# Turning the first expert stage's hidden rows in 32 by 32 blocks on VectorE, with weight sets released in two steps

## The reference, cut to what matters

```python
expert_idx = np.argmax(x @ w_gate, axis=1)      # 8 experts
for e in range(8):
    xe = x[expert_idx == e]
    h = np.maximum(xe @ w1[e], 0.0)             # 512 -> 1024
    out[mask] = gate_w[mask, None] * (h @ w2[e])  # 1024 -> 512
```

## Time and profile before

| | us |
|---|---|
| three runs | 1193.3, 1193.42, 1194.82 |
| median | 1193.42 |
| the profiled execution's own time | 1194.6 |
| its span | 1193.0 |
| PE busy | 1129.5 (95%) |
| DVE busy | 704.5 (59%) |
| ACT busy | 583.6 (49%) |
| POOL busy | 257.4 (22%) |

### The profile page before, as it was taken

The page is one execution under the profiler, slowest core; times in us unless marked ns, Lnnn a source line. Parts: engine busy times, 40 slices in busy tenths (PEclk is TensorE's granted clock), DMA queues, the critical chain, the costliest instruction groups (busy, mean ns, idle before and its releaser), DMA issues.

```text
span 1193.0 us, 19326 instructions
## 1 busy us (share of the span) xinstructions
PE 1129.5 (95%) x6205; PEld 930.1 (78%) x6206; DVE 704.5 (59%) x1373; ACT 583.6 (49%) x1041; POOL 257.4 (22%) x184
## 2 busy tenths in 40 slices
PE   5999899839999999999999999999999999999996
PEld 4777777738888888888887787888888888888885
DVE  5788788741111111111124997986986986986974
ACT  5767576512222222222234765665665665665662
POOL 1101111135255646637250000100100100100101
PEclk9999899969999999999999999999999999999999
DMA  9997851157377767858473001001001001000000
GB/s 184 304 223 180 213 139 57 43 196 248 116 255 229 246 221 248 262 179 284 157 274 126 1 1 37 36 1 36 35 0 36 35 0 36 35 0 1 36 1 35
DMA packets 138136, 141.44 MB, mean 119 GB/s; under 512 B 100448, under 2 KB 100448, under 8 KB 137056
## 3 DMA queue, kind: packets, MB, share of 16 engines
q0 software_dynamic: 27584, 92.48, 22.5%
q1 hardware_dynamic: 110496, 48.26, 16.2%
HBM read 117.65 MB, written 23.32 MB: 118 GB/s over the span
## 4 chain that ended last, share of the span: by engine, by line
PE 79%; DVE 12%; issue 3%; ACT 3%; DMA 2%; POOL 1%; SPq 0%; POOLq 0%; DVEq 0%; ACTq 0%
PE bank L955 21%; PE bank L957 21%; PE bank L956 21%; PE bank L806 3%; PE bank L843 3%; PE bank L819 2%; PE bank L986 2%; PE bank L787 2%; PE bank L859 2%; DVE poly L1499 1%; DVE gl L1521 1%; DVE poly L1497 1%; PE bank L950 1%; DVE prob L1166 1%; DVE quot_b L1491 1%
## 5 line engine op out<-in xcount | busy, mean ns | idle before, releaser
L441 POOL TENSOR_TENSOR w_lo<-stage,w_hi 128x2048 fp32r<-128x2048 f32 x32 | 147.3, 4603 | 55.5 <-DMA w_hi<-in_moe_w_dram 18.2
L955 PE MATMUL bank<-w_hi,gh 128*128 128x512 f32 x384 | 150.6, 392 | 2.4 <-DVE gl L1521 2.4
L955 PE MATMUL bank<-x2Th,w_hi 128*128 128x512 f32 x384 | 149.6, 390 | 1.9 <-ACT ybuf L666 1.4
L957 PE MATMUL bank<-w_hi,gl 128*128 128x512 f32 x384 | 149.5, 389 | 0.0
L956 PE MATMUL bank<-w_lo,gh 128*128 128x512 f32 x384 | 149.4, 389 | 0.0
L957 PE MATMUL bank<-x2Th,w_lo 128*128 128x512 f32 x384 | 149.4, 389 | 0.0
L956 PE MATMUL bank<-x2Tl,w_hi 128*128 128x512 f32 x384 | 149.4, 389 | 0.0
L558 POOL DMA_INDIRECT out_dram<-stage,ids x24 | 28.5, 1187 | 521.8 <-ACT stage L746 504.9
L1414 DVE TENSOR_TENSOR hTl<-bank,hTh 128x512 fp32r<-128x512 f32 x62 | 39.9, 685 | 151.8 <-ACT hTh L671 151.8
L1408 DVE TENSOR_TENSOR xTl<-bank,xTh 128x512 fp32r<-128x512 f32 x31 | 21.4, 691 | 159.3 <-ACT xTh L659 159.3
L955 PE MATMUL bank<-w_hi,xTh 128*128 x248 | 100.2, 404 | 2.3 <-DVE xTl L1408 1.6
(11 more groups left out here) (204 smaller groups left out, 2325.6 us busy)
## 6 DMA issues: line engine op xcount, KB each, us to landing
w_hi<-in_moe_w_dram POOLq DMA_DIRECT2D x32, 1024.0 KB, 5.9
stage<-in_moe_w_dram POOLq DMA_DIRECT2D x32, 1024.0 KB, 8.2
xg<-routed_x SPq DMA_DIRECT2D x31, 256.0 KB, 2.7
routed_y<-ybuf SPq DMA_DIRECT2D x31, 256.0 KB, 5.4
x<-routed_y SPq DMA_DIRECT2D x6, 1056.0 KB, 5.1
kraw<-in_k_dram SPq DMA_DIRECT2D x24, 256.0 KB, 4.3
qraw<-in_q_dram SPq DMA_DIRECT2D x24, 256.0 KB, 5.1
vraw<-in_v_dram SPq DMA_DIRECT2D x24, 256.0 KB, 5.6
```

What stands on the lines that cost most here:

```text
L441: pool.tensor_tensor(w_lo[:, at:at + CH], stage[:, c % 2, :], w_hi[:, at:at + CH].bitcast(F32), ALU.subtract).then_inc(chunk_ready, 1)
L955: pe.matmul(dst, lhs_hi, rhs_hi, start=first, stop=False)
L957: return pe.matmul(dst, lhs_lo, rhs_hi, start=False, stop=last)
```

## The change

It takes the eight transposes of `hbuf` away from PE for tiles 0 to 29. DVE turns `hbuf` instead, in blocks of 32 by 32, into a tile `hT` in SBUF (it lies where `poly` of the dense layer lies). One instruction reads 32 partitions and 8 blocks of 32 columns and writes 32 partitions, and 16 of them turn a tile, eight (`turn_h(t, 0)`) for rows 0 to 63 and eight for rows 64 to 127. DVE's x step of the next tile stands between the two groups. `hTh` and `hTl` are formed from `hT` in two halves by rows instead of from the PSUM banks in two halves by columns. The last tile is turned on PE as before. PE's up has two new waits: before it writes a bank of `H_ps`, the Relu of the tile before has read it. ACT's Relu has one: `hbuf` has been turned.

POOL's wait before a set is cut in two. `up_free` waits on `h_ps` for the up product of the last tile of the old expert, `down_free`, behind the first split, on `tile_done` for the down product.

```diff
-            def half_free(e):
-                n = pool.value_load(end_i[0:1, ds(e, 1)], min_val=1, max_val=MT + 1)
+            def up_free(e):
+                n = pool.value_load(end_i[0:1, 1, ds(e, 1)], min_val=2, max_val=2 * MT)
+                pool.wait_ge(h_ps, n)
+                settle(pool)
+            def down_free(e):
+                n = pool.value_load(end_i[0:1, 0, ds(e, 1)], min_val=2, max_val=MT + 1)
                 pool.wait_ge(tile_done, n)
                 settle(pool)

+                if old is not None:
+                    up_free(old)
                 cast_in(0, par, srcs, kinds)
                 cast_in(1, par, srcs, kinds)
                 for c in range(4):
                     split(s, c, par)
+                    if c == 0 and old is not None:
+                        down_free(old)
                     if c < 2:
                         cast_in(c + 2, par, srcs, kinds)

             def moe_ht(t):                                   # ACT
-                for n in range(2):
-                    act.wait_ge(ht_ps, 2 * t + n + 1)
-                    act.activation(hTh[:, 4 * n:4 * n + 4, :], HT_ps[n][:, :].rearrange("p (j n) -> p j n", j=4),
-                                   ACT.Copy).then_inc(ht_hi, 1)
+                for k in range(2):
+                    cols = slice(64 * k, 64 * k + 64)
+                    act.wait_ge(h_turned, 2 * t + k + 1)
+                    act.activation(hTh[:, :, cols], hT[:, :, cols], ACT.Copy).then_inc(ht_hi, 1)

                 for n in range(2):                           # PE, moe_up
+                    if not isinstance(t, int) or t > 0:
+                        pe.wait_ge(h_sb, 2 * t + n - 1)

                 moe_down(t - 1, off_down, e_down)            # PE, pe_tile
-                moe_turn_h(t)
                 moe_up(t + 1, off_up, e)

+            def turn_h(t, k):                                # DVE
+                if not isinstance(t, int) and k == 0:
+                    dve.wait_ge(ht_lo, 2 * t)
+                dve.wait_ge(h_sb, 2 * t + 2)
+                for q in (2 * k, 2 * k + 1):
+                    for r in range(4):
+                        rows = hbuf[q * QD:(q + 1) * QD, :].rearrange("p (j r i) -> p j r i", r=4, i=QD)[:, :, r, :]
+                        ins = dve.transpose(hT[r * QD:(r + 1) * QD, :, q * QD:(q + 1) * QD], rows)
+                ins.then_inc(h_turned, 1)

             def moe_ht(t):                                   # DVE
-                    dve.tensor_tensor(hTl[:, 4 * n:4 * n + 4, :], HT_ps[n][:, :].rearrange("p (j n) -> p j n", j=4),
-                                      hTh[:, 4 * n:4 * n + 4, :].bitcast(F32), ALU.subtract).then_inc(ht_lo, 1)
+                    dve.tensor_tensor(hTl[:, :, cols], hT[:, :, cols], hTh[:, :, cols].bitcast(F32),
+                                      ALU.subtract).then_inc(ht_lo, 1)

-            with dve.Fori(0, MT - 1) as t:
-                moe_x(t + 1); moe_ht(t)
+            turn_h(0, 0); moe_x(1); turn_h(0, 1); moe_ht(0)
+            with dve.Fori(1, MT - 1) as t:
+                turn_h(t, 0); moe_x(t + 1); turn_h(t, 1); moe_ht(t)
```

More of the change, by code:

```diff
@@ L18 @@
 E, F = 8, 1024
+QD = 32
 F2 = 2048
@@ L96, in build_program @@
         dest_i = keep("dest_i", [P, MT], I32)
-        end_i = keep("end_i", [P, E], I32)
+        end_i = keep("end_i", [P, 2, E], I32)
         last_at = keep("last_at", [P, E + 1])
@@ L160, in build_program @@
         x2Tl = over("x2Tl", [P, KB, G * P], F32R)
+        poly_at = free[1]
         poly = over("poly", [P, 2, G * P])
+        hT, _ = place("hT", [P, FB, P], F32, poly_at)
         quot_b = over("quot_b", [P, 2, G * P])
@@ L208, in build_program @@
         xg_in = [sem("xg_in0"), sem("xg_in1")]; xg_ps = sem("xg_ps"); xg_hi = sem("xg_hi"); xg_lo = sem("xg_lo")
-        h_ps = sem("h_ps"); h_sb = sem("h_sb"); ht_ps = sem("ht_ps"); ht_hi = sem("ht_hi"); ht_lo = sem("ht_lo")
+        h_ps = sem("h_ps"); h_sb = sem("h_sb"); ht_ps = sem("ht_ps"); h_turned = sem("h_turned"); ht_hi = sem("ht_hi"); ht_lo = sem("ht_lo")
         tile_done = sem("tile_done"); y_sb = sem("y_sb"); y_out = sem("y_out")
@@ L464, in cast_in, with weight_set @@
                     .then_inc(hi_in[c], 16)
-            def weight_set(s, par, srcs, kinds, next_srcs, next_kinds):
+            def weight_set(s, par, srcs, kinds, next_srcs, next_kinds, old=None):
+                if old is not None:
+                    up_free(old)
                 cast_in(0, par, srcs, kinds)
@@ L538, in _ @@
                     e = 2 * ep + par
[L539 to L546, removed]
+                    weight_set(e, par, expert_src(e), XK, expert_src(e + 1), XK, e - 2)
+            weight_set(E - 2, 0, expert_src(E - 2), XK, expert_src(E - 1), XK, E - 4)
+            weight_set(E - 1, 1, expert_src(E - 1), XK, w_in_src, ["w_in"] * 4, E - 3)
+            weight_set(E, 0, w_in_src, ["w_in"] * 4, w_out_src, ["w_out"] * 4, E - 2)
             for c in (2, 3):
@@ L649, in _, with moe_h @@
                     act_full(b)
-            def moe_h(t):
+            def moe_h(t, first=False):
                 for n in range(2):
                     act.wait_ge(h_ps, 2 * t + n + 1)
+                    if n == 0 and not first:
+                        act.wait_ge(h_turned, 2 * t)
                     act.activation(hbuf[:, n * 512:(n + 1) * 512], H_ps[n][:, :], ACT.Relu).then_inc(h_sb, 1)
@@ L668, in moe_ht, with last_ht @@
             def moe_ht(t):
+                for k in range(2):
+                    cols = slice(64 * k, 64 * k + 64)
+                    act.wait_ge(h_turned, 2 * t + k + 1)
+                    act.activation(hTh[:, :, cols], hT[:, :, cols], ACT.Copy).then_inc(ht_hi, 1)
+            def last_ht():
                 for n in range(2):
-                    act.wait_ge(ht_ps, 2 * t + n + 1)
+                    act.wait_ge(ht_ps, n + 1)
                     act.activation(hTh[:, 4 * n:4 * n + 4, :], HT_ps[n][:, :].rearrange("p (j n) -> p j n", j=4),
@@ L674, in _ @@
             moe_x(0)
-            moe_h(0); moe_x(1); moe_ht(0)
+            moe_h(0, True); moe_x(1); moe_ht(0)
             moe_h(1); moe_x(2); moe_y(0, True); moe_ht(1)
@@ L696, in _ @@
             split_high(1)
-            moe_y(MT - 2); moe_ht(MT - 1)
+            moe_y(MT - 2); last_ht()
             x2_high(0, 1, first_ps)
@@ L980, in moe_down, with last_turn_h @@
                 mm.then_inc(tile_done, 1)
-            def moe_turn_h(t):
+            def last_turn_h():
                 for n in range(2):
-                    pe.wait_ge(h_sb, 2 * t + n + 1)
+                    pe.wait_ge(h_sb, 2 * (MT - 1) + n + 1)
                     for j in range(4):
@@ L1001, in _ @@
             moe_turn_x(1, 1)
-            moe_turn_h(0)
             moe_up(1, off, e)
@@ L1025, in _ @@
             moe_down(MT - 2, off_down, e_down)
-            moe_turn_h(MT - 1)
+            last_turn_h()
             turn_x2(0, 1, first_ps)
@@ L1403, in _ @@
             tl(dve.tensor_scalar(edge[:, 1, :], tile_end[:, :], 1.0, None, ALU.add))
-            dve.tensor_copy(end_i[:, :], edge[:, 1, :]).then_inc(tab_ready, 1)
+            tl(dve.tensor_scalar(edge[:, 2, :], tile_end[:, :], 2.0, None, ALU.mult))
+            dve.tensor_copy(end_i[:, :, :], edge[:, 1:3, :]).then_inc(tab_ready, 1)
             def moe_x(t):
@@ L1409, in moe_x, with last_ht @@
                                   ALU.subtract).then_inc(xg_lo, 1)
-            def moe_ht(t):
+            def turn_h(t, k):
[7 more added lines that the diff above has]
+                ins.then_inc(h_turned, 1)
+            def moe_ht(t):
+                for k in range(2):
+                    cols = slice(64 * k, 64 * k + 64)
+                    dve.wait_ge(ht_hi, 2 * t + k + 1)
+                    dve.tensor_tensor(hTl[:, :, cols], hT[:, :, cols], hTh[:, :, cols].bitcast(F32),
+                                      ALU.subtract).then_inc(ht_lo, 1)
+            def last_ht():
                 for n in range(2):
-                    dve.wait_ge(ht_hi, 2 * t + n + 1)
+                    dve.wait_ge(ht_hi, 2 * (MT - 1) + n + 1)
                     dve.tensor_tensor(hTl[:, 4 * n:4 * n + 4, :], HT_ps[n][:, :].rearrange("p (j n) -> p j n", j=4),
@@ L1482, in _ @@
             split_low(1)
-            moe_ht(MT - 1)
+            last_ht()
             x2_low(0, 1, first_ps)
```

## The result

The changed kernel is slower: 1212.55 us in the median (1210.82 to 1216.58) against 1193.82 before, a ratio of 1.0156 with a 95% interval of 1.0132 to 1.0181. The forecast was 1172.3 in a range of 1166 to 1206. The sign was wrong, and the time lies outside the range. The mechanism is that of rival 1: the difference meets the splits. The profiled execution took 1210.82 us, its span is 1209.2.

A forecast was written before the change was run, and what follows sets the result against it. PE's instructions bound the expert stage. Shorter rounds -25.2, start +2.7, end wait +1.4 make -21.1 us on 1194.6, so 1173.5, or 1172.3 in the median; range 1166 to 1206, the forecast's own 1168 to 1177.

The forecast's parts named there:

- rival 1: Differences forming `hTl`, now with two SBUF inputs, wait out POOL's splits: 2.6 to 4.9 us a set, 1199 us; chance 0.35.
- the price of the difference with its new operand: DVE's differences forming `hTl` from SBUF: 1.29 us for both as before, nothing added in the sum.
- The round with POOL idle: PE's time from one turning of x to the next: 11.4 us instead of 12.29, 0.87 less a tile.
- The transpose: Each DVE transpose of `hbuf`, 32 partitions by 256 elements: 0.43 us, with ends of 0.29 and 0.69.
- rival 2: DVE's transposes are slow, 0.69 us each, and DVE becomes the bound: 1220 us; chance 0.11.
- The wait before `turn_x2`: At the end of the expert stage, PE waits for DVE's gate steps queued behind `hTl` of 29: new, 1.4 us.
- The edit of the release alone: POOL's wait before a weight set cut in two: worth 0, as PE waits for no weights.
- the count of waits: PE's waits on `hTl` if differences meet splits: 14 to 20 times.
- Its sign in the profile: If differences meet splits, DVE idles in front of the difference until a split ends.
- The start: At tile 0, up(1) waits behind eight DVE transposes: cost 2.7 us, PE idle some 4.5.
- the clock: After PE's idle time at the start, another fall of the clock: up to 1.7 us, none taken in the sum.

The follow-up runs named there:

- e1: Changed kernel with the block-turned rows in two PSUM banks instead of SBUF: 1174.69 us, ratio 0.9848 against the kernel before.
- e3: Kernel before with only the release in two steps, rows still turned on TensorE: 1193.47 against 1193.38 us, ratio 1.0002.
- e6: Changed kernel with each GpSimd split cut in four pieces of 512 columns, no wait between: 1221.04 us, ratio 1.0228 against the kernel before.
- e2: Changed kernel with the old release, one wait before a weight set: 1202.83 us, ratio 1.0082 against the kernel before.
- e9: Changed kernel with each split in four pieces, GpSimd waiting for each piece's end before the next: 1177.73 us, ratio 0.9859 against the kernel before.
- e5: Kernel before plus three VectorE operations a tile on a constant (copy, transpose, difference, SBUF to SBUF): 1193.54 us in one run.
- e10: Turned rows in PSUM, tile 0 on TensorE, gate steps early, but with the old release: 1173.34 us, ratio 0.9822 against the kernel before.

## Why the prediction was wrong

**The step that failed** is the price of the difference with its new operand. I priced it at nothing in the sum, because `hTl` had never taken over 692 ns beside splits. But that row is of a difference with one input in PSUM; it says nothing of one with two in SBUF, as the prediction itself noted under rival 1. In its place the runs showed a difference that waits out a split (up to 5.28 us for one of 0.69, 18 times) and PE waiting 28.5 us for it. The e1 run settles it: the same edit with the turned rows in PSUM gives 1174.7, which is 2.4 above the forecast of 1172.3, about what the start cost beyond its forecast.

**What was right.** The round with POOL idle, 11.4 forecast and 11.36 measured. The transpose, 0.43 and 0.436; rival 2 is out. The estimate from the Trainium skill ("VectorE: DVE Perf Modes", The three transpose paths), 0.44, was as good, and the trace agrees with it. The wait before `turn_x2`, 1.4 and 1.6. The edit of the release alone is worth 0 (e3). Rival 1's mechanism, and the count of waits (14 to 20, found 17). Its sign in the profile was wrong, though: VectorE was expected to idle in front of the difference, and the trace books the time as busy. And "for the whole instruction", as rival 1 has the exclusion, is too short for the cut splits of e6, where 14 times in 20 it lasted over four instructions.

**What was mis-sized.** Rival 1: 2.6 to 4.9 us a set were forecast. The 28 rounds took 354.63, where 28 x 11.36 = 318.1 would be free of it, so 36.5 us or 5.2 a set. PE's waits are 28.5 of them, 4.1 a set, within the forecast. Two things come on top that the rival didn't have. The two falls of the clock behind a wait cost some 3 us (PE is busy for 13.24 us in such a round and for 11.62 in one with a wait alone). And each of the 17 waits costs another 0.24: PE's busy time in such a round is 11.61 instead of 11.37, as the first product no longer starts over the end of the transposes. The start: 2.7 forecast, 5.9 measured. PE was idle for 4.7, as forecast, but the clock cost 2.4, which the prediction had put at up to 1.7 and kept for the range only. So rival 1 as it happened is 1193.4 - 25.7 for the 28 rounds + 36.5 + 5.9 + 0.4 at the end = 1210.5, near the measured 1212.6. The stated range ended at 1206, below the rival's own 1209, and rival 1 had no fall of the clock in it.

**The choice among the cases.** Rival 1 had 0.35. The one new fact about the operation was its operands, and no row spoke against the rule that rival 1 took for them; there was no row of the trace in its favour either.

**The release** was priced at 0 and was so alone (e3), but not together with the new operand: 1202.8 without it and 1212.6 with it (e2).

## What to carry to other kernels

When an edit moves an operand of a VectorE operation from PSUM to SBUF, look at what GpSimd reads at that time: a row of the same operation with a PSUM operand is no price for it. In a trace the hold shows as a long maximum on a line with a constant median, booked as busy, with an end that follows the end of the GpSimd operation by a constant time. A free PSUM bank for the intermediate removes it (1174.7 us here), and where there is none, pieces on GpSimd with an idle moment between them (1177.7).

## What the runs showed of the hardware that I had not expected

- GpSimd can keep the access over instructions queued back to back (5.8 us for four pieces of 1.3, in 14 of 20 splits of e6), and gives it up in a gap of 0.18 us every time (e9).
- It holds the other way too. A piece of GpSimd that stands behind a difference takes 1.74 us instead of 1.29 (e6), and a split whose record starts while a difference runs takes 5.07 instead of 4.6 (e2, at 342.90).
- A copy with one SBUF input and an SBUF output is held like a difference with two, up to 4.7 us for one of 0.42 (e5).
- An operation of 32 columns, 0.19 us long, can be held for 4.4 us (e10). Size is no protection.
- VectorE writes block transposes straight into a PSUM bank, at 0.457 us against 0.436 into SBUF (e1).
- PE's clock can fall behind waits of 2.15 us where PE was otherwise busy: the two rounds of 15.39 us. But other waits of the same kernel, up to 2.31 us, had no fall behind them, and with the same number of waits e6 had seven falls; what decides it stays open.
